# A fused linear attention, routing and expert kernel: prologue and routing reordered beside the attention step, with filler products

## What is computed

```python
def _attn_ref(r, k, v, w, u):          # (B, H, S, D) = (4, 8, 768, 48)
    for t in range(S):
        cur = np.einsum('bhd,bhe->bhde', u[None] * kt, vt)
        y[:, :, t] = np.einsum('bhd,bhde->bhe', rt, state + cur)
        state = wt[:, :, :, None] * state + np.einsum('bhd,bhe->bhde', kt, vt)

def _moe_ref(x, expert_emb, tau, w1, w2):   # x (3072, 384), 8 experts, hidden 1024
    logits = xn @ en.T / tau                # rows of x and of expert_emb divided by their norms
    expert_idx = np.argmax(logits, axis=1)  # gate_w: softmax probability of that expert
    for e in range(E):
        h = np.maximum(x[mask] @ w1[e], 0.0)
        out[mask] = gate_w[mask, None] * (h @ w2[e])

def _moe2_ref(x, w1, w2, w3, w_out):        # hidden 768
    h = np.maximum(np.maximum(x @ w1, x @ w2), x @ w3)
    return h @ w_out
```

## Time and profile before

| | |
|---|---|
| median of 3 runs | 777.75 us (777.35 to 778.68) |
| profiled execution | 777.89 us, span 776.2 us |
| TensorE busy | 720.7 us, 93% of the span |
| VectorE, ScalarE, GpSimd busy | 417.3, 300.7, 129.0 us |
| mean granted TensorE clock | 0.967 of 2.4 GHz |

### The profile page before, as it was taken

How to read it: one execution, slowest core, us unless ns; L and a number is a source line. 1 busy time by engine, 2 the same in 40 slices (tenths; PEclk the granted TensorE clock), 3 DMA queues, 4 the chain that set the end, 5 groups by cost and what they waited for, 6 DMA issues and landing times.

```text
span 776.2 us, 13361 instructions
## 1 busy us (share of the span) xinstructions
PE 720.7 (93%) x5026; PEld 648.4 (84%) x5026; DVE 417.3 (54%) x659; ACT 300.7 (39%) x616; POOL 129.0 (17%) x121
## 2 busy tenths in 40 slices
PE   4599999999338999999999999999999999999995
PEld 3598999998228999999999998898898988988885
DVE  6688888887665666565445444423324233243231
ACT  4266666665225556555435544202202022021120
POOL 3534433340134232000000000010020110200102
PEclk9699999999759999999999999999999999999999
DMA  9988878951037575543343340000010000100001
GB/s 143 157 155 141 138 133 135 150 132 33 17 102 238 163 223 162 157 122 106 99 133 110 93 130 0 1 27 15 1 41 1 20 21 1 41 0 11 32 0 41
DMA packets 148683, 66.49 MB, mean 86 GB/s; under 512 B 119560, under 2 KB 146320, under 8 KB 148624
## 3 DMA queue, kind: packets, MB, share of 16 engines
q1 hardware_dynamic: 132752, 51.44, 30.8%
q0 software_dynamic: 3072, 9.54, 3.3%
q10 hardware_dynamic: 12800, 4.72, 2.6%
HBM read 56.14 MB, written 9.54 MB: 85 GB/s over the span
## 4 chain that ended last, share of the span: by engine, by line
PE 90%; DVE 3%; issue 3%; DMA 1%; POOL 1%; SPq 1%; ACT 1%; DVEq 0%; POOLq 0%; ACTq 0%
PE bank L1319 22%; PE bank L1321 22%; PE bank L1320 22%; PE bank L1347 4%; PE bank L1360 3%; PE bank L1425 3%; PE bank L1400 3%; PE bank L1405 3%; PE bank L1415 3%; PE bank L1380 2%; PE bank L1370 1%; DMA x_got<-x_tokens,slot_tok 1%; PE bank L1485 1%; DVE low_hot L1140 1%; POOL rku L560 0%
## 5 line engine op out<-in xcount | busy, mean ns | idle before, releaser
L1319 PE MATMUL bank<-bh,mh 128*128 128x512 f32 x324 | 127.4, 393 | 0.0
L1321 PE MATMUL bank<-bh,ml 128*128 128x512 f32 x324 | 126.7, 391 | 0.0
L1320 PE MATMUL bank<-bl,mh 128*128 128x512 f32 x324 | 125.7, 388 | 0.0
L623 POOL DMA_INDIRECT out_dram<-o_put,slot_tok x24 | 25.2, 1052 | 440.3 <-DVE o_put L1289 440.3
L1298 DVE TENSOR_TENSOR g<-bank,g 128x512 f32<-128x512 f32 x36 | 24.9, 692 | 122.6 <-ACT g L847 122.6
L1240 DVE SCALAR_TENSOR_TENSOR hl<-bank,hh 128x432 fp32r<-128x432 f32 x64 | 38.9, 607 | 77.6 <-ACT hh L802 73.2
L1319 PE MATMUL bank<-xh,w1h 128*128 128x432 f32 x192 | 71.8, 374 | 2.2 <-DVE xl L1193 2.2
L1321 PEld LDWEIGHTS bank<-bh,ml 128*128 128x128 f32 x324 | 60.6, 187 | 14.3
L1320 PEld LDWEIGHTS bank<-bl,mh 128*128 128x128 f32 x324 | 60.8, 188 | 13.1
L1319 PEld LDWEIGHTS bank<-bh,mh 128*128 128x128 f32 x324 | 60.9, 188 | 12.4
L847 ACT COPY g<-bank 128x512 f32<-128x512 f32 x36 | 21.1, 587 | 126.9 <-PE bank L1321 126.9
(11 more groups left out here) (191 smaller groups left out, 1395.3 us busy)
## 6 DMA issues: line engine op xcount, KB each, us to landing
w_raw<-in_moe_w_dram SPq DMA_DIRECT2D x79, 384.0 KB
raw_w<-in_w_dram SPq DMA_DIRECT2D x32, 144.0 KB, 4.1
raw_k<-in_k_dram SPq DMA_DIRECT2D x32, 144.0 KB, 4.4
raw_r<-in_r_dram SPq DMA_DIRECT2D x32, 144.0 KB, 4.5
vals<-in_v_dram SPq DMA_DIRECT2D x32, 144.0 KB, 3.4
x_tokens<-x_rows ACTq DMA_DIRECT2D x32, 144.0 KB, 3.8
w_raw<-in_moe_w_out_dram SPq DMA_DIRECT2D x3, 384.0 KB
x_got<-x_tokens,slot_tok POOLq DMA_INDIRECT x24
```

Of the source, the lines that this page charges most:

```text
L623: pool.indirect_dma_start(out=out, out_offset=bass.IndirectOffsetOnAxis(ap=slot_tok[:, n:n + 1], axis=0), in_=o_put[:, n % SB, :], in_offs ...
L1319: pe.matmul(dst, sh, mh_, start=first, stop=False)
L1320: pe.matmul(dst, sh, ml_, start=False, stop=False)
L1321: return pe.matmul(dst, sl_, mh_, start=False, stop=last)
```

## The change

The file is changed in four places.

- **The start.** The embeddings' loads and `k` of unit 0 are issued on ScalarE's queue; `u` has a semaphore of its own (`u_in`). GpSimd makes `ident` first. VectorE and ScalarE do the embeddings' arithmetic ahead of unit 0's first running product, with one load of ScalarE's table. `own_of(0)` stands behind `mask(0, 0)`, `own_of(1)` behind `mask(0, 1)` and the filling of `to_rows`. TensorE makes 36 products of a tile of ones before the first load arrives, and 10 more behind the first turn.
- **The batches.** `add_dots` stands ahead of `keys_of`, with the first two operations on the batch's best experts behind it (`largest_of`) and, one unit later, the other three (`first_of`).
- **The routing.** Only the last batch is left at the end. `hot` and `earlier` are bfloat16. One running sum over all experts and tiles replaces the sum by expert and the offsets. ScalarE makes the half of `high_parts` that GpSimd made. The list comes from 48 products of 24 columns, accumulated in one place, and `slot_tok` is written ahead of the table. 28 filler products follow the list and 4 each flip.
- **Slot 0.** Weight chunks 4 and 5 have room of their own (`w_more`) and are loaded during attention. `xh` and `xl` of slot 0 are split tile by tile from PSUM (`first_x`, `first_low`). The last columns of `xs` are cleared behind the fourth gather, the tile of a step is flipped one step later, and ScalarE copies `slot_dots`.

```diff
-                        sp.dma_start(emb_in[:, :], emb).then_inc(small_in, 16)
-                        sp.dma_start(tau_col[:, :], tau.rearrange("(a b) -> a b", a=1).broadcast_to([P, 1])
-                                     ).then_inc(small_in, 16)
...
+            act.dma_start(emb_in[:, :], emb).then_inc(small_in, 16)
...
+            for i in range(2):
+                act.dma_start(raw["k"][:, 0, :, i, 0:D], k[0, i].rearrange("(c q) d -> q c d", q=P)
+                              ).then_inc(raw_in["k"][0], 16)
+            act.wait_ge(warm_ok, 1)
+            act.activation(squares[:, 0:1], ones[0:E, 0:1], ACT.Sqrt).then_inc(act_seq, 1)
+            act.wait_ge(small_in, 32)
...
-            for c in range(WRAW):
+            for c in range(EARLY):
                 first_chunk(c)
...
             pool.wait_ge(suffix_ok, 2)
-            for n in range(2):
-                own_products(n)
-                own_times_u(n)
+            own_products(0)
+            own_times_u(0)
+            own_products(1)
             own_values(0)
+            own_times_u(1)
...
-            pool.memset(xs[:, :, SLOT + N:], 0.0).then_inc(pad_ok, 1)
-
-            pool.wait_ge(placed, 1)
-            pool.tensor_tensor(out=high_parts[:, :, 0, :], in0=high_hot[:, :, :],
-                               in1=parts[:, :, 0].unsqueeze(2).broadcast_to([P, NT, NT]), op=ALU.mult
-                               ).then_inc(numbered, 1)
...
+            act.activation(high_parts[:, :, 0, :], high_hot[:, :, :], ACT.Copy, scale=tok_low[:, 0:1]
+                           ).then_inc(numbered, 1)
...
+            def first_x(t):
+
+                width = min(P, SLOT - P * t)
+                src = bank[t % 2][:, 0:DM].rearrange("q (c t) -> q c t", c=KD)
+                act.wait_ge(x_flipped, t + 1)
+                act.copy(xh[:, :, P * t:P * t + width], src[:, :, 0:width]).then_inc(xh_ok, 1)
+
             for t in range(reach(0)):
+                first_x(t)
                 square_tile(t)
...
+            def largest_of(b, after):
+                rows = slice(CH * b, CH * (b + 1))
+                dve.wait_ge(dots_ok, b + 1)
+                after(dve.tensor_reduce(out=best[:, :], in_=dots[:, rows, :], axis=AX, op=ALU.max))
+                after(dve.tensor_tensor(maxed[:, :, :], dots[:, rows, :],
+                                        best[:, :].unsqueeze(2).broadcast_to([P, CH, E]), ALU.is_equal))
...
+                if n > 1 and n % PAIRS == 0:
+                    add_dots(n // PAIRS - 1)
+                    largest_of(n // PAIRS - 1, after)
+                if n > PAIRS and n % PAIRS == 1:
+                    first_of(n // PAIRS - 1, after)
                 if n + 1 < ALL:
                     keys_of(n + 1)
...
+            dve.wait_ge(hots, 1)
+            mark(dve.tensor_copy(count[:, 0:1], cum[:, 0:1, NT - 1]))
+            mark(dve.tensor_tensor(count[:, 1:], cum[:, 1:, NT - 1], cum[:, 0:E - 1, NT - 1], ALU.subtract))
+            dve.tensor_copy(slot_tok[:, :], bank[0][:, 0:NT]).then_inc(listed, 1)
...
+            pe.wait_ge(warm_ok, 1)
+            for _ in range(START_WARM):
+                pe.matmul(bank[7][:, 0:P], ones[:, :], ones[:, :], start=True, stop=True)
...
-                    if f < len(tiles):
-                        flip(tiles[f])
+                    if 1 <= f <= len(tiles):
+                        flip(tiles[f - 1])
```

More of the change, by code:

```diff
@@ L83, in linear_attention_moe_max_mlp @@
     later = sb("later", [P, HALF, P])
-    all_ones = sb("all_ones", [P, P])
-    earlier = sb("earlier", [P, P])
+    all_ones = sb("all_ones", [P, NT * E])
+    earlier = sb("earlier", [P, P], BF16)
+    ones = sb("ones", [P, P], BF16)
+    hot = sb("hot", [P, E, NT], BF16)
+    best, lead = sb("best", [P, CH]), sb("lead", [P, CH])
+    maxed = sb("maxed", [P, CH, E])
+    iota_slot = sb("iota_slot", [P, SLOTS + 1])
+    iota_lim = sb("iota_lim", [P, LIMS])
     u_row = sb("u_row", [P, H, 64])
@@ L322, in landed, with raw_chunk @@
             return rest % WRAW, 16 * (len(ALONE) // WRAW) * s + 16 * (rest // WRAW + 1)
+        def raw_chunk(s, c):
+            b, _ = landed(s, c)
+            return w_more[:, c - WRAW] if isinstance(s, int) and s == 0 and WRAW <= c < EARLY else w_raw[:, b]
+        MORE = (SLOT + P - 1) // P - KD
         def late_landed(n, x):
@@ L898, in embeddings, with rows_matrix @@
                 dve.tensor_scalar(emb_in[:, :], emb_in[:, :], emb_s[:, 7:8], None, ALU.mult).then_inc(emb_unit, 1)
+            def rows_matrix():
+                dve.wait_ge(consts, 1)
                 dve.wait_ge(emb_turned, 1)
+                for i in range(2):
+                    rows = slice(64 * i, 64 * i + D)
+                    mark(dve.tensor_copy(to_rows[rows, :, D * i:D * (i + 1)],
+                                         ident[rows, rows].unsqueeze(1).broadcast_to([D, PAIRS, D])))
+                settle()
                 for i in range(2):
@@ L1427, in rows_of @@
                 ins.then_inc(x_turned, 1)
-            for name in "wkr":
-                turn_raw(0, name)
+            turn_raw(0, "w")
+            for _ in range(NEXT_WARM):
+                pe.matmul(bank[7][:, 0:P], ones[:, :], ones[:, :], start=True, stop=True)
+            embeddings()
+            turn_raw(0, "k")
+            turn_raw(0, "r")
             turn_raw(1, "w")
@@ L1465, in _ @@
             pe.matmul(bank[0][:, 0:NT * E], earlier[:, :], flat, start=True, stop=True)
[L1466 removed]
+            pe.matmul(bank[1][:, 0:NT * E], ones[:, :], flat, start=True, stop=True).then_inc(counted, 1)
             pe.wait_ge(numbered, 2)
@@ L1471, in _, with stay_warm @@
                     pe.wait_ge(low_made, m // (NT // 4) + 1)
-                ins = pe.matmul(bank[0][:, 0:LISTED * NT], low_hot[:, m, :],
-                                high_parts[:, m, :, :].rearrange("q x c -> q (x c)"), start=(m == 0),
-                                stop=(m == NT - 1))
+                for x in range(LISTED):
+                    ins = pe.matmul(bank[0][:, 0:NT], low_hot[:, m, :], high_parts[:, m, x, :],
+                                    start=(m == 0 and x == 0), stop=(m == NT - 1 and x == LISTED - 1))
             ins.then_inc(hots, 1)
+            def stay_warm(times):
+                for _ in range(times):
+                    pe.matmul(bank[7][:, 0:NT * E], ones[:, :], flat, start=True, stop=True)
+            stay_warm(LIST_WARM)
             pe.wait_ge(table, 1)
```

235 lines of the change are left out of this document (117 added, 118 removed).

## The result

The changed kernel takes 758.12 us (median of 4 runs, 757.63 to 759.66); the kernel before, measured together with it, 777.55 us (776.52 to 778.68). The ratio is 0.9753, with a 95% interval of 0.9733 to 0.9774. The profiled execution took 757.63 us, its span 755.9 us, 20.3 us less than before, at a mean granted clock of 0.981.

A forecast was written before the change was run, and what follows sets the result against it. TensorE holds 90% of the last-ending chain, so only its waits and slow clock in start, routing and slot 0 could pay. 9.0 − 0.4 + 12.1 = 20.7 us off 777.9 gave 757.2, range 751.5 to 763.5.

The forecast's parts named there:

- Start: Stretch before `scores(1, 0)`: reordered loads and five-engine chain bring it from 39.21 to 30.3, called 9.0 us earlier.
- Batches: Attention units: batch work in front of `keys_of` loses 0.4 us over six units, bounds 0 to 1.5.
- the 1.57 us of `rec_s`: Batch's last unit: `rec_s` ready at 80.19, taken by TensorE at 81.76; 1.57 us cover against about 1.0 us of work.
- Routing to `slot_tok`: Routing after attention: `slot_tok` written at 210.7 against 217.01, with the gather starting 6.4 us earlier.
- Gathers and slot 0: From routing through slot 0's first `down`: 12.1 us saved in all, including the routing's 6.4.
- Of the clock half was counted as won: Slot 0's first stretch: half clock costs 3.2 us; fillers fill only between waits, so 1.6 us counted.
- a clock above 0.8: Expected profile sign in slot 0, where the clock before was 0.72 over 11.45 us.
- TensorE at half clock in slot 0: Rival in slot 0: half clock stays and gathers land late, losing 3 to 4 us: 760.7; chance 0.15.
- its late landing: Part of the slot 0 half-clock rival: gathers land late, costing 1.0 us; the forecast took 3.0 us for landing.
- the third rival: Attention batches: VectorE work outruns its cover, TensorE stalls and drops to half clock, losing 24.6 us: 781.5; chance 0.02.

The follow-up runs named there:

- own_first: Changed kernel with the order of `own_of` and GpSimd's products in unit 0 as before the change; median 760.19 us.
- more_fill: Changed kernel with 28 filler products instead of 4 behind the flip of tile 2 in slot 0; median 758.06 us.
- spread: Changed kernel with a batch's work divided over four units, `add_dots` behind `suffix_of`; median 758.53 us.
- batch_behind: Changed kernel with the batches' VectorE work moved from in front of `keys_of` to behind `suffix_of`; median 761.46 us.
- gp_parts: Changed kernel with one half of `high_parts` made by GpSimd instead of ScalarE; median 760.02 us.
- low_behind: Changed kernel with all six `low_chunk` operations of slot 0 behind the loop over its first four tiles; median 756.92 us.

## Why the prediction was right

The forecast was 757.2 us, measured 758.12, for the reasons given in most parts.

- **Start, forecast 9.0 us, measured 9.1.** The chain was as described: `rec_s` at 13.44 (forecast 13.8), GpSimd at 15.36 (16.1), `mix_state` at 27.95 (28.2). Two of its steps were off and cancel, which is luck: `prefix_of(1)` started at 23.65, not 24.8, and took 0.9 us longer than priced, since it met GpSimd's product. own_first shows the new order worth 2.55 us up to `prefix_of(1)`, and 1.6 once this meeting is paid.
- **Batches, forecast 0.4 us lost, measured 1.5.** This term was mis-sized, and its cover misread. `rec_s` never became late. The prediction had named the mask as the one that slips, at 0.1 to 0.2 us, and units 5, 9 and 13 lost 0.3 to 0.4 and the units behind them 0.1 to 0.2. It took the 1.57 us of `rec_s` for the cover; the mask had 0.87 us. And it lacked the shared port. The later running product delays GpSimd, and `own_values` then meets VectorE's prefix step. Ahead of the three larger waits the meeting is at L951, 0.58 to 0.70 us instead of 0.17; ahead of the three smaller ones at the scan, 0.64 us longer. more_fill's unit 5 has the work without the meeting and loses nothing; spread has meetings with the work in pieces and loses 0.2; batch_behind, with the same work in another place, loses 2.6.
- **Routing to `slot_tok`, forecast 6.3 us, measured 6.4.** VectorE's five operations took 1.16 us (1.2), the branch 0.8 (0.4), TensorE's products 0.5 (0.4), a piece of `low_hot` 0.87 to 0.89 (0.86). gp_parts confirms the 1.1 us ascribed to GpSimd's product with 0.96.
- **Gathers and slot 0, forecast 12.1 us with the routing, measured 12.5** (down at 221.24 against 241.75, less 7.56 of attention and 0.5 for the flip that moved). The fourth gather's issue ended 6.4 us behind `slot_tok` (6.5) and landed 3.2 us later (3.0). TensorE has no idle time between slot 0's first product and `down`, as forecast. Of the clock half was counted as won: a stretch at half clock was left from 214.4 to 217.7, 1.65 us lost (1.6). That this fits so well is luck in part, since this stretch differs between profiles, from 5.70 to 7.26 us with the same fillers and code. The sign that was named, a clock above 0.8, was missed (0.76).
- **The rivals.** TensorE at half clock in slot 0 came true only by the half that was counted in the forecast; its late landing did not (3.2 us, forecast 3.0). Of the third rival the batches showed the mechanism without a fall of the clock: 1.5 us lost in the units, not 24.6. That the start's clock would differ between executions was in none of them: the profiled execution was one that escaped, and the median is 0.5 us above it. Whether unit 1 is the reason for that half microsecond isn't shown, for the other runs have no profile.

## What to carry to other kernels

Where two engines share a port, price a moved operation by what the other engine does at its new place: here operations of 0.2 us took 0.2 or, in another place, 0.9 or 1.2 us. A wait of TensorE that costs nothing on the path can still cost clock behind it, in some executions and not in others. One profile can't price such a thing: compare with profiles of kernels whose edit lies elsewhere, as the unit 1 and slot 0 columns allow here. Fillers belong in such waits (40 in front of `mix_state(0)`, two of two profiles without a loss) and brought nothing where VectorE sets the time (36 at the start). Small work beside a loop that TensorE bounds is free only in pieces below the cover of each round, and the cover is that of the operation with the least of it: 1.0 us in one unit cost up to 0.4 against the mask's 0.87, the same in four pieces almost nothing.

## What the runs showed of the hardware

- VectorE operations with two SBUF inputs and GpSimd's products, which read SBUF, exclude one another for whole operations, both ways: a scan of 1.77 us took 2.68, `own_v` of 1.15 us took 2.61, a product of 0.21 us on 48 elements 1.19. The Trainium skill, "SBUF — State Buffer", section "SBUF: two separate sides", describes this as an exclusive lock; the traces agree.
- One small VectorE operation with a single SBUF input waits too: L951 (128x6) took 0.5 to 1.1 us where `own_v` had started before it, instead of 0.17, ending 0.02 to 0.03 us behind it (0.58 us at 66.14 in the changed kernel).
- A gather's issue on GpSimd waits for such an operation too: 1.29 and 1.43 us beside `low_chunk`, ending 0.87 us behind the end of one of its pieces (206.83 and 208.57), and 1.00 without (low_behind). That is against what the same page of the Trainium skill, "SBUF — State Buffer", infers under "Who interferes with whom", that such an operation leaves descriptor writing alone.
- A gathered tile landed later beside a weight load. In the changed kernel the second and the third tile were turned 2.1 us behind their issue's end and the fourth, with a weight load issued at 208.75, 3.2 us; in low_behind, with no such load, the fourth took 2.1. That the load is the cause was not tested by itself.
- TensorE's idle time in front of `mix_state(0)`, 1.9 to 3.6 us, was followed by half clock (1.2 GHz) in unit 1 in nine of eleven profiles, at a cost of 0.5 to 3.2 us; in the other two (3.16 and 3.31 us idle) unit 1 ran at full clock (2.4 GHz). With 40 products in it, 1.3 us idle, there was no loss in two of two profiles.
